# Routed expert items: where two steps of the second layer stand, and first-layer weights split in four pieces

## The chip, the cores and the metric

The kernel runs on one core of one Trainium2 chip. The metric is the device time of one execution in microseconds (us), from the program's first to its last instruction with what lies around it. Engines are named as the profile names them: PE is TensorE (PEld its weight loads), DVE is VectorE, ACT is ScalarE, POOL is GpSimd, SP is the engine that issues the large loads.

## The reference

Three parts follow one another: clustered attention, a mixture of eight experts in which every token goes to one expert, and a second, dense mixture whose eight experts see every token. The change touches the middle part only. N is 1536 tokens, D 512, F 1024, E 8 experts; everything is 32-bit floating point.

```
def _moe_ref(x, expert_emb, tau, w1, w2):
    xn = x / (norm(x) + 1e-06); en = expert_emb / (norm(expert_emb) + 1e-06)
    logits = xn @ en.T / tau
    expert_idx = argmax(logits, axis=1)
    probs = softmax(logits);  gate_w = probs[arange(N), expert_idx]
    for e in range(E):
        mask = expert_idx == e
        h = maximum(x[mask] @ w1[e], 0.0)          # first layer, relu
        out[mask] = gate_w[mask, None] * (h @ w2[e])   # second layer
```

## The kernel before

A product of 32-bit numbers is made from three faster ones. Each operand is split in a high part (fp32r, written by ACT, `split_hi`, line 877, the instruction at L879) and a low part (written by DVE, `split_lo`, line 882, the instruction at L884, which subtracts the high part from the operand). PE then adds high by high, high by low and low by high.

The routed part sorts the tokens by expert and cuts them in 19 items of 128 tokens; item n has one expert. Items 0 and 1 are written out (`tile(0, 0)`, `tile(0, 1)`), items 2 to 17 are a hardware loop of two items a turn, item 18 has a code of its own (`last_tile`) that also begins the dense part. Each engine runs its own program; what couples them are semaphores, and what stands in an engine's queue behind a waiting instruction waits with it.

For an item PE does this (`tile`, line 1253): the first layer's output half s = 0 in 12 products (lines 1267 to 1269), half s = 1 in 12 products with the four transposes of the first hidden half in their middle (`transpose_h(n, 0)`, L1217), then the four transposes of the next item's tokens (`transpose_x`, L1210), the four of the second hidden half (`transpose_h(n, 1)`, L1217), and the second layer in eight steps f = 0 to 7 of three products each (lines 1280 to 1282). Steps 0 to 3 read the first hidden half and the first half of w2, steps 4 to 7 the second halves.

Between them stand, for every item:

- ACT: `read_out` of the item before (L1528), the high part of the second half of w2 (`w2_part(.., 1)`), the relu of each hidden half (L1506), the high parts of the hidden halves (`h_part`), of the next tokens (`x_part`), of the next item's w1 in the pieces of `W1_PARTS`, and of the next item's first half of w2.
- DVE: the low parts of the same data: w2's second half, first hidden half, tokens, second hidden half, w1's pieces, w2's first half. It reads the item's expert number into a register ahead of w1's pieces (`expert_of`, L1801).
- POOL: adds the item before to the output rows (`add_rows`, L2167) and then gathers the tokens of the item after next with an indirect DMA (`gather`, L2124).
- SP: loads the raw weights of an expert a good item ahead of their use.

Weights are split anew for every item: w1 is 128 x 4096 numbers, w2 the same.

What the names in the profile are: `moe_bank` is PSUM; `all_w_hi`, `all_w_lo`, `all_w_raw` are w1; `moe_routed_w_hi`, `moe_routed_w_lo`, `moe_w_raw` are w2; `moe_h_rows` is the relu's output, `moe_routed_h_hi` and `moe_routed_h_lo` the transposed hidden halves; `moe_x_rows` the gathered tokens and `moe_x_hi`, `moe_x_lo` their transposes; `all_x` holds the output rows, `moe_y` one item's output.

Of the kernel before, what the change touches and what calls it, by code (L numbers as in the profile page):

```python
# [24 lines left out]
W1_PARTS = ((0, 2, 0), (2, 2, 0), (0, 4, 1))  # L25
# [155 lines left out]
def attention(nc, sems, c, made, q, k, v, centroids, expert_emb, tau, w1, X, L, xs, W1R, w1_loaded, x_stored):  # L181
# [7 lines left out]
    with ExitStack() as stack:  # L189
# [346 lines left out]
        def scalar(act, experts):  # L536
# [89 lines left out]
            experts.first_w1_hi(act, 2)  # L626
            copy_out_t(G // 2 - 1, 13)
# [277 lines left out]
def expert_layers(nc, sems, attn, c, X, L, w1, w2, xs, out_row, w_gate, dense_w1, dense_w2, out_dram, W1R, W1H, W1L,  # L905
                  w1_at, stationary_at, scratch_at, w1_loaded, x_stored):

    with ExitStack() as stack:
# [291 lines left out]
        def tensor(pe):  # L1200
# [52 lines left out]
            def tile(i, j):  # L1253
# [3 lines left out]
                for s in range(2):  # L1257
                    pe.wait_ge(w1_lo, 3 * n + s + 2)
# [14 lines left out]
                if not last:  # L1273
                    transpose_x(i + j, 1 - j)
                transpose_h(n, 1)
                for f in range(FC):
                    if f % 4 == 0:
                        pe.wait_ge(rh_lo, 2 * n + f // 4 + 1)
                        pe.wait_ge(rw2_lo, 2 * n + f // 4 + 1)
                    pe.matmul(ps_y[:], RHH[:, f, :], RW2H[:, f, :], start=(f == 0), stop=False)  # L1280
                    pe.matmul(ps_y[:], RHH[:, f, :], RW2L[:, f, :], start=False, stop=False)  # L1281
                    mm = pe.matmul(ps_y[:], RHL[:, f, :], RW2H[:, f, :], start=False, stop=(f == FC - 1))  # L1282
                    if f == 3:
                        mm.then_inc(w2_used, 1)
# [189 lines left out]
        def scalar(act):  # L1474
# [55 lines left out]
            def tile(i, j):  # L1530
# [13 lines left out]
                h_part(n, 0)  # L1544
                relu(n, 1)
                x_part(n + 1)
                h_part(n, 1)
                if first:
                    r = expert_of(n + 1)
                    w1_part(i + j, 1 - j, 0, r)  # L1550
                w1_part(i + j, 1 - j, 1, r)
                w1_part(i + j, 1 - j, 2, r)
# [205 lines left out]
        def vector(dve):  # L1758
# [44 lines left out]
            def w1_part(n, r, part):  # L1803
                dve.wait_ge(w1_hi, 3 * n + part + 1)
# [80 lines left out]
            def tile(i, j):  # L1885
# [4 lines left out]
                if first:  # L1890
                    sum_gates()
                    h_part(n, 0)
                    w2_part(n, 0, 1)
                else:
                    w2_part(n, expert_of(n), 1)
                    h_part(n, 0)
                x_part(n + 1)
                h_part(n, 1)
                if first:
                    find_gates()  # L1900
                r = expert_of(n + 1)
                w1_part(n + 1, r, 0)
                w1_part(n + 1, r, 1)
                w1_part(n + 1, r, 2)
# [194 lines left out]
            first_w1_lo(dve, 2)  # L2099
            w2_part(0, 0, 0)  # L2100
# [199 lines left out]
```

## Time and profile before

| | us |
|---|---|
| median of three runs | 1614.45 (1612.37 to 1615.25) |
| the profiled execution's own time | 1614.62 |
| its span | 1612.8 |
| granted clock of TensorE over the span | 0.994 |
| items 2 to 17 (351.47 to 557.01) | 16 times 12.85 |

The page of the profile gives PE 1578.4 us of busy time (98% of the span), DVE 1189.9 (74%), ACT 771.0 (48%), POOL 247.2 (15%). In the stretch of the routed items, which lies between 323 and 579 us, DVE stands near PE. A row of a timeline gives the start of an instruction in us, its duration in us, engine, line, operation, and in square brackets the idle time of the engine before it with what ended that idle time. Instructions of an engine overlap a little: the next DVE instruction starts some 0.08 us before the row's end of the one ahead, and a matmul's row lasts 0.39 us while the next one starts 0.23 us after it.

### The profile page before, as it was taken

The page shows a single profiled execution, that of the slowest core. Times are in us where ns is not written, and L with a number is a line of the kernel's source. Part 1 is how long each engine was busy: PE and PEld are TensorE (multiplying, and loading weights), DVE is VectorE, ACT ScalarE, POOL GpSimd, SP SyncE. Part 2 cuts the span into 40 slices and gives each one's busy share as a digit, 9 for nine tenths or more (in the row PEclk, how much of TensorE's full clock was granted, in tenths as well). Part 3 has the DMA queues.
Part 4 walks back from the last instruction along what each step waited for, and adds up shares of the span by engine and source line. Part 5 has one row for each costly group of instructions (what it writes and reads, how often), then busy time and mean ns, then how long its engine had stood idle before and what let it go on. Part 6 is the DMA issues. An engine that isn't in the chain of part 4 may idle for free.

```text
span 1612.8 us, 27116 instructions
## 1 busy us (share of the span) xinstructions
PE 1578.4 (98%) x8416; PEld 1397.6 (87%) x8416; DVE 1189.9 (74%) x2010; ACT 771.0 (48%) x1377; POOL 247.2 (15%) x314
## 2 busy tenths in 40 slices
PE   8999999899999989999999999999999999999998
PEld 7999999677777778898998989899898989989897
DVE  7999999999999974877665666656566665656664
ACT  5777779778888852322333233233323323222331
POOL 2111111213333350100010010001001000100102
PEclk8999999999999999999999999999999999999999
DMA  4223323354334310110010011001001100100002
GB/s 100 60 60 71 76 59 89 92 190 145 141 130 141 132 40 14 40 40 27 27 53 26 26 39 40 26 26 53 26 26 40 39 26 27 52 26 26 26 0 78
DMA packets 123699, 94.91 MB, mean 59 GB/s; under 512 B 66344, under 2 KB 101160, under 8 KB 123632
## 3 DMA queue, kind: packets, MB, share of 16 engines
q1 hardware_dynamic: 120848, 86.01, 17.7%
q0 software_dynamic: 2480, 8.13, 1.7%
q8 instruction: 21, 0.34, 0.1%
q14 instruction: 46, 0.38, 0.1%
q10 hardware_dynamic: 304, 0.05, 0.0%
HBM read 87.88 MB, written 6.29 MB: 58 GB/s over the span
## 4 chain that ended last, share of the span: by engine, by line
PE 88%; DVE 7%; issue 3%; ACT 2%; DMA 0%; DVEq 0%; SPq 0%; POOL 0%; ACTq 0%; POOLq 0%
PE moe_bank L1346 11%; PE moe_bank L1344 11%; PE moe_bank L1345 11%; PE moe_bank L1321 10%; PE moe_bank L1324 10%; PE moe_bank L1323 10%; PE attn_ps_out L441 2%; PE moe_bank L1267 2%; PE moe_bank L1269 2%; PE moe_bank L1268 2%; PE attn_ps_probs_t L422 2%; PE moe_bank L1280 2%; PE moe_bank L1282 2%; PE moe_bank L1281 2%; PE attn_ps_prep L347 1%
## 5 line engine op out<-in xcount | busy, mean ns | idle before, releaser
L1968 DVE SCALAR_TENSOR_TENSOR all_x<-moe_bank,all_x 128x512 f32<-128x512 f32 x336 | 251.3, 748 | 129.1 <-PE moe_bank L1346 126.4
L1321 PE MATMUL moe_bank<-moe_x_t_hi,all_w_hi 128*128 128x384 f32 x896 | 305.1, 341 | 3.0 <-DVE all_w_lo L884 2.9
L1324 PE MATMUL moe_bank<-moe_x_t_hi,all_w_lo 128*128 128x384 f32 x896 | 303.2, 338 | 0.0
L1323 PE MATMUL moe_bank<-moe_x_t_lo,all_w_hi 128*128 128x384 f32 x896 | 302.3, 337 | 0.0
L1344 PE MATMUL moe_bank<-moe_w_hi,moe_h_hi 128*128 128x512 f32 x768 | 301.1, 392 | 0.0
L1345 PE MATMUL moe_bank<-moe_w_lo,moe_h_hi 128*128 128x512 f32 x768 | 300.8, 392 | 0.0
L1346 PE MATMUL moe_bank<-moe_w_hi,moe_h_lo 128*128 128x512 f32 x672 | 265.0, 394 | 0.0
L1321 PEld LDWEIGHTS moe_bank<-moe_x_t_hi,all_w_hi 128*128 128x128 f32 x896 | 168.6, 188 | 14.0 <-issue 3.6
L1323 PEld LDWEIGHTS moe_bank<-moe_x_t_lo,all_w_hi 128*128 128x128 f32 x896 | 168.6, 188 | 11.3
L1324 PEld LDWEIGHTS moe_bank<-moe_x_t_hi,all_w_lo 128*128 128x128 f32 x896 | 168.5, 188 | 0.0
L1345 PEld LDWEIGHTS moe_bank<-moe_w_lo,moe_h_hi 128*128 128x128 f32 x768 | 144.2, 188 | 22.4
L1344 PEld LDWEIGHTS moe_bank<-moe_w_hi,moe_h_hi 128*128 128x128 f32 x768 | 144.4, 188 | 21.8
L2129 POOL TENSOR_TENSOR moe_w_sums<-moe_dense_w_raw 128x256 f32<-128x256 f32 x32 | 23.7, 740 | 853.0 <-DVE all_w_lo L884 853.0
L1346 PEld LDWEIGHTS moe_bank<-moe_w_hi,moe_h_lo 128*128 128x128 f32 x672 | 126.0, 188 | 28.6
L1676 ACT ACTIVATE moe_h_hi<-all_x 128x384 fp32r<-128x384 f32 x63 | 33.2, 526 | 169.4 <-DVE all_x L2077 169.4
L1648 ACT ACTIVATE moe_h_hi<-moe_p 128x384 fp32r<-128x384 f32 x63 | 33.2, 526 | 147.0 <-DVE moe_p L2036 147.0
L2036 DVE TENSOR_TENSOR moe_p<-moe_bank,moe_p 128x384 f32<-128x384 f32 x63 | 35.1, 557 | 90.7 <-PE moe_bank L1324 80.2
L884 DVE TENSOR_TENSOR moe_routed_w_lo<-moe_w_raw,moe_routed_w_hi 128x2048 fp32r<-128x2048 f32 x38 | 98.7, 2598 | 4.5 <-ACT moe_routed_w_hi L879 3.7
L637 DVE TENSOR_TENSOR attn_probs_t_lo<-attn_ps_probs_t,attn_probs_t_hi 128x384 fp32r<-128x384 f32 x192 | 97.1, 546 | 2.4 <-ACT attn_probs_t_hi L564 1.3
L1669 ACT ACTIVATE moe_h_hi<-moe_bank 128x384 fp32r<-128x384 f32 x63 | 31.0, 492 | 134.6 <-PE moe_bank L1324 134.6
L691 DVE CUSTOM_DVE_ANT_0 attn_scores<-attn_ps_scores,attn_mask 128x768 f32<-128x768 f32 x96 | 91.1, 949 | 2.6 <-issue 0.6
L558 ACT ACTIVATE attn_probs<-attn_scores,attn_row_max 128x768 f32<-128x768 f32 x96 | 91.3, 951 | 3.2 <-DVE attn_row_max L691 3.1
(325 smaller groups left out, 3065.7 us busy)
## 6 DMA issues: line engine op xcount, KB each, us to landing
all_w_raw<-in_moe_w SPq DMA_DIRECT2D x8, 2048.0 KB, 7.5
moe_w_raw<-in_moe_w SPq DMA_DIRECT2D x8, 2048.0 KB, 9.2
moe_dense_w_raw<-in_moe_w SPq DMA_DIRECT2D x64, 256.0 KB, 3.1
moe_dense_w_raw<-in_moe_w SPq DMA_DIRECT2D x32, 512.0 KB, 3.3
attn_q_raw<-in_q SPq DMA_DIRECT2D x32, 192.0 KB, 3.4
attn_k_raw<-in_k SPq DMA_DIRECT2D x32, 192.0 KB, 3.8
attn_v_raw<-in_v SPq DMA_DIRECT2D x16, 192.0 KB, 3.8
tokens<-all_x SPq DMA_DIRECT2D x32, 96.0 KB, 2.0
```

Source lines behind the costliest of these rows:

```text
L558: act.activation(PR[s % 2][:], SM[s % 2][:], ACT.Exp, bias=MX[s % 2][:], scale=-1.0, accum_out=SUM[:, s % 12:s % 12 + 1]).then_inc(exp_don ...
L637: return dve.tensor_tensor(out, src, hi.bitcast(F32), ALU.subtract)
L691: dve.tensor_tensor_reduce(out=SM[s % 2][:].rearrange("p (a k) -> p a k", a=2), in0=ps_s[s % 2][:, :, 0:3 * P], in1=MASK[s % 2][:].rearran ...
L884: return dve.tensor_tensor(out, src, hi.bitcast(F32), ALU.subtract)
L1321: pe.matmul(out, hi[:, s, k, :], XH[chunk][:, x, k, :], start=(start and k == 0), stop=False, skip_group_check=True)
L1323: pe.matmul(out, hi[:, s, k, :], XL[chunk][:, x, k, :], start=False, stop=False, skip_group_check=True)
L1324: mm = pe.matmul(out, lo[:, s, k, :], XH[chunk][:, x, k, :], start=False, stop=(stop and k == 1), skip_group_check=True)
L1344: pe.matmul(out, HH[h][hidden][:, rows], W2H[j][:, f, :], start=(f == 0), stop=False)
L1345: pe.matmul(out, HH[h][hidden][:, rows], W2L[j][:, f, :], start=False, stop=False)
L1346: mm = pe.matmul(out, HL[h][hidden][:, rows], W2H[j][:, f, :], start=False, stop=(f == 1))
L1968: dve.scalar_tensor_tensor(acc, y, PROB[:, row, bass.ds(at, 1)], acc, ALU.mult, ALU.add).then_inc(y_added, 1)
L2036: dve.tensor_tensor(CP1[:], m, CP1[:], ALU.add).then_inc(summed, 1)
```

## The change

In PE's queue the first two steps of the second layer (f = 0, 1) come ahead of the transposes of the second hidden half, and these ahead of the transposes of the next tokens; item 18 has the first of these moves too. w1 is split in four pieces of 128 x 1024 in place of two of 128 x 1024 and one of 128 x 2048, also for the first weights, which are prepared during the attention part. From item 1 on, DVE makes the first two of these pieces between the two hidden halves, then the second hidden half, the tokens and the other two pieces; ACT makes the pieces 1 and 2 on either side of the second relu, and the second hidden half ahead of the tokens. The semaphore counts follow (four pieces an item).

```diff
--- before.py
+++ after.py
@@ -22,7 +22,7 @@
 DC, FC = D // P, F // P
 ITEMS = NT + E - 1
 FOLD = DH + E
-W1_PARTS = ((0, 2, 0), (2, 2, 0), (0, 4, 1))
+W1_PARTS = ((0, 2, 0), (2, 2, 0), (0, 2, 1), (2, 2, 1))
 ROUNDS = 8
 
 
@@ -624,6 +624,7 @@
             for s in range(2, 12):
                 step(G // 2 - 1, s)
             experts.first_w1_hi(act, 2)
+            experts.first_w1_hi(act, 3)
             copy_out_t(G // 2 - 1, 13)
 
         def rank(engine, done):
@@ -1255,7 +1256,7 @@
                 last = last_of(i, j)
                 pe.wait_ge(rx_lo, n + 1)
                 for s in range(2):
-                    pe.wait_ge(w1_lo, 3 * n + s + 2)
+                    pe.wait_ge(w1_lo, 4 * n + 2 * s + 2)
                     if first_of(i) and j == 1 and s == 1:
                         find_gates()
                     for k in range(DC):
@@ -1270,10 +1271,11 @@
                     mm.then_inc(h_ready, 1)
                     if last:
                         transpose_pair(2 * s)
-                if not last:
-                    transpose_x(i + j, 1 - j)
-                transpose_h(n, 1)
                 for f in range(FC):
+                    if f == 2:
+                        transpose_h(n, 1)
+                        if not last:
+                            transpose_x(i + j, 1 - j)
                     if f % 4 == 0:
                         pe.wait_ge(rh_lo, 2 * n + f // 4 + 1)
                         pe.wait_ge(rw2_lo, 2 * n + f // 4 + 1)
@@ -1542,14 +1544,18 @@
                     act.wait_ge(found, SCALED)
                     read_out(0, 0)
                 h_part(n, 0)
+                if not first:
+                    w1_part(i + j, 1 - j, 1, r)
                 relu(n, 1)
+                if not first:
+                    w1_part(i + j, 1 - j, 2, r)
+                h_part(n, 1)
                 x_part(n + 1)
-                h_part(n, 1)
                 if first:
                     r = expert_of(n + 1)
-                    w1_part(i + j, 1 - j, 0, r)
-                w1_part(i + j, 1 - j, 1, r)
-                w1_part(i + j, 1 - j, 2, r)
+                    for part in range(3):
+                        w1_part(i + j, 1 - j, part, r)
+                w1_part(i + j, 1 - j, 3, r)
                 w2_part(i + j, 1 - j, 0, r)
                 if not first:
                     if not first_of(i):
@@ -1801,7 +1807,7 @@
                 return dve.value_load(expert[0:1, bass.ds(n, 1)], min_val=0, max_val=E - 1)
 
             def w1_part(n, r, part):
-                dve.wait_ge(w1_hi, 3 * n + part + 1)
+                dve.wait_ge(w1_hi, 4 * n + part + 1)
                 chunk, chunks, s = W1_PARTS[part]
                 cols = slice(s * 512, (s + 1) * 512)
                 split_lo(dve, W1L[:, chunk:chunk + chunks, cols], W1R[:, bass.ds((r % 2) * DC + chunk, chunks), cols],
@@ -1891,17 +1897,22 @@
                     sum_gates()
                     h_part(n, 0)
                     w2_part(n, 0, 1)
+                    h_part(n, 1)
+                    x_part(n + 1)
+                    find_gates()
+                    r = expert_of(n + 1)
+                    for part in range(4):
+                        w1_part(n + 1, r, part)
                 else:
                     w2_part(n, expert_of(n), 1)
                     h_part(n, 0)
-                x_part(n + 1)
-                h_part(n, 1)
-                if first:
-                    find_gates()
-                r = expert_of(n + 1)
-                w1_part(n + 1, r, 0)
-                w1_part(n + 1, r, 1)
-                w1_part(n + 1, r, 2)
+                    r = expert_of(n + 1)
+                    w1_part(n + 1, r, 0)
+                    w1_part(n + 1, r, 1)
+                    h_part(n, 1)
+                    x_part(n + 1)
+                    w1_part(n + 1, r, 2)
+                    w1_part(n + 1, r, 3)
                 w2_part(n + 1, r, 0)
                 if first:
                     dve.wait_ge(gates_found, 1)
@@ -2097,6 +2108,7 @@
             shift_logits()
             x_part(0)
             first_w1_lo(dve, 2)
+            first_w1_lo(dve, 3)
             w2_part(0, 0, 0)
             turns(dve, tile)
             first_unit()
```

PE's queue in a loop item, from the last product of the first layer on, before (`moe_h_relu` is the relu of a hidden half, `moe_x_loaded` a gather's landing, `moe_routed_w2_lo` and `moe_routed_h_lo` are DVE's low parts):

```order
L1269 MATMUL moe_bank<-all_w_hi,moe_x_lo 128x512
L1210 MATMUL moe_bank<-all_ident,moe_x_rows 128x128 [waits moe_x_loaded0]
L1210 MATMUL moe_bank<-all_ident,moe_x_rows 128x128 x3
L1217 MATMUL moe_bank<-all_ident,moe_h_rows 128x128 [waits moe_h_relu]
L1217 MATMUL moe_bank<-all_ident,moe_h_rows 128x128 x3
L1280 MATMUL moe_bank<-moe_routed_w_hi,moe_routed_h_hi 128x512 [waits moe_routed_w2_lo,moe_routed_h_lo]
L1281 MATMUL moe_bank<-moe_routed_w_lo,moe_routed_h_hi 128x512
L1282 MATMUL moe_bank<-moe_routed_w_hi,moe_routed_h_lo 128x512
L1280 MATMUL moe_bank<-moe_routed_w_hi,moe_routed_h_hi 128x512
```

and now, from the same product on (line numbers are one or two higher):

```order
L1270 MATMUL moe_bank<-all_w_hi,moe_x_lo 128x512
L1282 MATMUL moe_bank<-moe_routed_w_hi,moe_routed_h_hi 128x512 [waits moe_routed_w2_lo,moe_routed_h_lo]
L1283 MATMUL moe_bank<-moe_routed_w_lo,moe_routed_h_hi 128x512
L1284 MATMUL moe_bank<-moe_routed_w_hi,moe_routed_h_lo 128x512
L1282 MATMUL moe_bank<-moe_routed_w_hi,moe_routed_h_hi 128x512
L1283 MATMUL moe_bank<-moe_routed_w_lo,moe_routed_h_hi 128x512
L1284 MATMUL moe_bank<-moe_routed_w_hi,moe_routed_h_lo 128x512
L1218 MATMUL moe_bank<-all_ident,moe_h_rows 128x128 [waits moe_h_relu]
L1218 MATMUL moe_bank<-all_ident,moe_h_rows 128x128 x3
L1211 MATMUL moe_bank<-all_ident,moe_x_rows 128x128 [waits moe_x_loaded0]
L1211 MATMUL moe_bank<-all_ident,moe_x_rows 128x128 x3
L1282 MATMUL moe_bank<-moe_routed_w_hi,moe_routed_h_hi 128x512
```

The two steps and their wait for DVE's low parts stand in front of both groups of transposes, which now follow one another.

DVE's queue in a loop item, from the second half of w2 on, before (rows that only compute a register are left out):

```order
L884 TENSOR_TENSOR moe_routed_w_lo<-moe_w_raw,moe_routed_w_hi 128x2048
L884 TENSOR_TENSOR moe_routed_h_lo<-moe_bank,moe_routed_h_hi 128x512 [waits moe_routed_h_hi]
L884 TENSOR_TENSOR moe_x_lo<-moe_bank,moe_x_hi 128x512 [waits moe_routed_x_hi]
L884 TENSOR_TENSOR moe_routed_h_lo<-moe_bank,moe_routed_h_hi 128x512 [waits moe_routed_h_hi]
L884 ISA [waits moe_w1_hi_done]
L884 TENSOR_TENSOR all_w_lo<-all_w_raw,all_w_hi 128x2x512
L884 ISA [waits moe_w1_hi_done]
L884 TENSOR_TENSOR all_w_lo<-all_w_raw,all_w_hi 128x2x512
```

and now:

```order
L885 TENSOR_TENSOR moe_routed_w_lo<-moe_w_raw,moe_routed_w_hi 128x2048
L885 TENSOR_TENSOR moe_routed_h_lo<-moe_bank,moe_routed_h_hi 128x512 [waits moe_routed_h_hi]
L885 ISA [waits moe_w1_hi_done]
L885 TENSOR_TENSOR all_w_lo<-all_w_raw,all_w_hi 128x2x512
L885 ISA [waits moe_w1_hi_done]
L885 TENSOR_TENSOR all_w_lo<-all_w_raw,all_w_hi 128x2x512
L885 TENSOR_TENSOR moe_routed_h_lo<-moe_bank,moe_routed_h_hi 128x512 [waits moe_routed_h_hi]
L885 TENSOR_TENSOR moe_x_lo<-moe_bank,moe_x_hi 128x512 [waits moe_routed_x_hi]
L885 ISA [waits moe_w1_hi_done]
L885 TENSOR_TENSOR all_w_lo<-all_w_raw,all_w_hi 128x2x512
L885 ISA [waits moe_w1_hi_done]
L885 TENSOR_TENSOR all_w_lo<-all_w_raw,all_w_hi 128x2x512
```

The item's order on DVE is now: first hidden half, two pieces of w1, second hidden half, tokens, two pieces of w1. What stands ahead of the first hidden half, w2's second half with its wait for ACT, has not moved.

## Rows read from the trace of the kernel before

**Rows 1.** Busy time of each engine over the stretch of items 2 to 17: us, PE, PEld, DVE, ACT, POOL.
```profile
351.00:557.00 206.00, 201.99 (x963) 163.85 (x962) 188.70 (x129) 175.31 (x177) 73.42 (x31) 1.00 0.42 147
```

**Rows 2.** Timeline of PE in items 8 and 9: start, us, line, operation.
```profile
428.55 0.40 PE L1267 MATMUL moe_bank<-all_w_hi,moe_x_hi 128*128 128x512 f32 x1
...
434.35 0.39 PE L1269 MATMUL moe_bank<-all_w_hi,moe_x_lo 128*128 128x512 f32 x1
...
435.43 0.66 PE L1217 MATMUL moe_bank<-all_ident,moe_h_rows 128*128 128x128 f32 x4 [0.25 <-ACT moe_h_rows L1506]
...
436.15 0.39 PE L1281 MATMUL moe_bank<-moe_routed_w_lo,moe_routed_h_hi 128*128 128x512 f32 x1
...
441.40 0.40 PE L1267 MATMUL moe_bank<-all_w_hi,moe_x_hi 128*128 128x512 f32 x1
```

**Rows 3.** Timeline of DVE in the same two items.
```profile
432.19 2.83 DVE L884 TENSOR_TENSOR moe_routed_w_lo<-moe_w_raw,moe_routed_w_hi 128x2048 fp32r<-128x2048 f32 x1 [0.48 <-ACT moe_routed_w_hi L879]
434.94 0.68 DVE L884 TENSOR_TENSOR moe_routed_h_lo<-moe_bank,moe_routed_h_hi 128x512 fp32r<-128x512 f32 x1
...
436.75 0.69 DVE L884 TENSOR_TENSOR moe_routed_h_lo<-moe_bank,moe_routed_h_hi 128x512 fp32r<-128x512 f32 x1 [0.16 <-ACT moe_routed_h_hi L879]
437.80 1.23 DVE L884 TENSOR_TENSOR all_w_lo<-all_w_raw,all_w_hi 128x1024 fp32r<-128x1024 f32 x1 [0.36 <-ACT all_w_hi L879]
...
442.28 2.28 DVE L884 TENSOR_TENSOR moe_routed_w_lo<-moe_w_raw,moe_routed_w_hi 128x2048 fp32r<-128x2048 f32 x1
444.64 3.22 DVE L884 TENSOR_TENSOR moe_routed_w_lo<-moe_w_raw,moe_routed_w_hi 128x2048 fp32r<-128x2048 f32 x1
```

**Rows 4.** Timeline of ACT, the second half of the second-layer weights.
```profile
430.03 1.92 ACT L879 ACTIVATE moe_routed_w_hi<-moe_w_raw 128x2048 fp32r x1 [0.45 <-issue]
...
442.48 1.92 ACT L879 ACTIVATE moe_routed_w_hi<-moe_w_raw 128x2048 fp32r x1
```

**Rows 5.** Timeline of POOL, items 8 and 9, then item 1.
```profile
430.89 1.97 POOL L2167 TENSOR_TENSOR all_x<-all_x,moe_y 128x512 f32 x1 [7.90 <-issue]
433.02 2.83 POOL L2124 DMA_INDIRECT moe_x_rows<-tokens,moe_token_of_item  x1 [0.15 <-POOL all_x L2167]
444.11 1.61 POOL L2167 TENSOR_TENSOR all_x<-all_x,moe_y 128x512 f32 x1 [8.26 <-issue]
...
344.98 1.27 POOL L2167 TENSOR_TENSOR all_x<-all_x,moe_y 128x512 f32 x1 [22.05 <-issue]
346.40 0.96 POOL L2124 DMA_INDIRECT moe_x_rows<-tokens,moe_token_of_item  x1
```

**Rows 6.** Timeline of DVE and PE where item 1 starts.
```profile
335.29 2.36 DVE L884 TENSOR_TENSOR all_w_lo<-all_w_raw,all_w_hi 128x1024 fp32r<-128x1024 f32 x2 [0.51 <-issue]
337.80 0.47 PE L1267 MATMUL moe_bank<-all_w_hi,moe_x_hi 128*128 128x512 f32 x1 [1.37 <-DVE all_w_lo L884]
```

**Rows 7.** Timeline of PE, eight transposes and what follows (item 18).
```profile
562.43 1.06 PE L1238 MATMUL moe_bank<-all_ident,moe_token_sums 128*128 128x128 f32 x8 [1.80 <-POOL moe_token_sums L2159]
563.25 0.48 PE L1267 MATMUL moe_bank<-all_w_hi,moe_x_hi 128*128 128x512 f32 x1
563.56 0.39 PE L1268 MATMUL moe_bank<-all_w_lo,moe_x_hi 128*128 128x512 f32 x1
```

**Rows 8.** Timeline of DVE in item 0.
```profile
328.95 0.69 DVE L884 TENSOR_TENSOR moe_routed_h_lo<-moe_bank,moe_routed_h_hi 128x512 fp32r<-128x512 f32 x1 [0.59 <-ACT moe_routed_h_hi L879]
...
332.95 0.16 DVE L1876 CAST moe_gate_part<-moe_gate 128x12 bf16<-128x12 f32 x1
```

**Rows 9.** Timeline of DVE and PE in item 1.
```profile
344.61 0.68 DVE L884 TENSOR_TENSOR moe_routed_h_lo<-moe_bank,moe_routed_h_hi 128x512 fp32r<-128x512 f32 x1
...
346.21 0.39 PE L1281 MATMUL moe_bank<-moe_routed_w_lo,moe_routed_h_hi 128*128 128x512 f32 x1
```

**Rows 10.** Timeline of PE behind its longest wait.
```profile
594.75 0.41 PE L1321 MATMUL moe_bank<-moe_x_t_hi,all_w_hi 128*128 128x384 f32 x1 [2.94 <-DVE all_w_lo L884]
...
596.61 0.52 PE L1321 MATMUL moe_bank<-moe_x_t_hi,all_w_hi 128*128 128x384 f32 x1
```

## The prediction

> **What bounds the kernel now.** I read the page first (PE busy 98% of the span, so only what lies on PE's own path can move the time), then the busy time by stretch, then the timelines of PE, DVE, ACT and POOL over two neighbouring loop items. In the stretch of items 2 to 17 DVE is busy 188.7 of 206 us and PE 202.0 [rows 1]: two engines near their limit. An item lasts 441.40 - 428.55 = 12.85 us [rows 2], and the 16 items of the loop are alike.
>
> I count times in an item from its first product (T = 428.55 for item 8, 441.40 for item 9). The last product of the first layer starts at 5.80. Then come the eight transposes, and the second product of the second layer starts at 7.60 [rows 2]: 1.80 us. Eight transposes without a gap take less: 0.23 to the first of them, 0.82 for the eight, 0.31 from the first product behind them to the second [rows 7], together 1.36. The missing 0.44 us is the hole in which PE waits for the relu; its row shows 0.25 of it as idle, the rest is the pipeline's emptying. That hole is what the change can remove: 16 x 0.44 = 7.0 us.
>
> The other side is what the first two steps need: DVE's low part of the first hidden half, which stands behind DVE's low part of w2's second half. It ends at 434.94 + 0.68 = 435.62 in item 8, T + 7.07, and at the same place in item 9 (444.64 + 3.22 = 447.86 ends w2, and the hidden half follows as in item 8) [rows 3]. PE could start the second layer at T + 6.03, so today these low parts come one microsecond too late for the new place; the transposes cover that now.
>
> **When the low part will be ready.** Call its end E. What sets it is w2's second half on DVE, so I take that apart.
>
> - ACT's high part of it ends at T + 3.40 in even items (430.03 + 1.92) and T + 3.00 in odd ones (442.48 + 1.92) [rows 4]. It cannot come earlier, since it waits for the item before to end and for its read-out. DVE begins 0.24 behind it (432.19 against 431.95) [rows 3, 4]: T + 3.64 and T + 3.24.
> - DVE's own queue is later than that now (w2's first half runs at T + 0.88 to 3.16 in item 9, 442.28 + 2.28 [rows 3]). With the new order it will not be: below, w2's first half ends near T + 2.0.
> - POOL's addition. It starts at T + 2.34 (430.89), lasts 1.97 there, but 1.27 in item 1, where DVE leaves it alone [rows 5]. In item 9 DVE's w2 starts at 444.64, takes 3.22 instead of 2.28, and ends 2.14 behind the addition's end (444.11 + 1.61 = 445.72); in item 8 it ends 435.02, 2.16 behind 432.86 [rows 3, 5]. So the two do not overlap: whichever comes second does its work behind the other. The Trainium skill says the same (SBUF — State Buffer, section Who interferes with whom): a DVE instruction with two inputs in SBUF and a GpSimd instruction that reads SBUF exclude one another for a whole instruction, and the loser waits. By that rule, which these rows bear out, the estimate for an odd item is the later one of the two that follow; if the two engines only overlapped freely, it would be the earlier one.
> - With DVE idle at T + 2.34 the addition runs alone and ends at T + 2.34 + 1.27 = 3.61. Odd items: DVE is blocked from 3.24 to 3.61, needs 2.15 more, 5.76; the hidden half starts 0.08 ahead of that row's end and lasts 0.68: E = T + 6.36. Even items: DVE starts at 3.64, lasts 2.28: E = 3.64 + 2.28 - 0.08 + 0.68 = T + 6.52. Without the blocking the odd ones would have E = 3.24 + 2.88 = T + 6.12.
>
> **The new item.** Behind a DVE end PE's first product starts 0.15 later (335.29 + 2.36 = 337.65 against 337.80 [rows 6]) and the second 0.31 after it, as behind transposes [rows 7]: E + 0.46. Today 5.25 us lie between the second product and the next item (441.40 - 436.15 [rows 2]), 23 spacings of 0.228. New: four spacings to the end of step 1 (0.91), 1.36 for the eight transposes up to the second product behind them, 17 spacings (3.88). So the item lasts E + 0.46 + 0.91 + 1.36 + 3.88 = E + 6.61. It breaks even at E = 6.24, and it is over that in both kinds: 12.97 in odd items, 13.13 in even ones, mean 13.05, against 12.85. That is +0.20 x 16 = **+3.2 us** where -7 was to be had.
>
> Is anything else later than E? The second hidden half: its transposes start at E + 1.37 + 0.23 = E + 1.60. Now it takes 436.75 - 435.43 = 1.32 from their start to DVE's low part [rows 2, 3], which gives E + 2.92, end E + 3.60, and 0.15 to PE: E + 3.75. Step 4 wants it at E + 0.46 + 0.91 + 1.36 + 5 x 0.228 = E + 3.87. It just fits. DVE is free for it: behind the first hidden half come 0.36 for reading the expert (437.80 row) and two pieces of w1, 2.36 in one row of two [rows 3, 6], to about E + 2.64. Then tokens (0.61), two pieces (2.28) and w2's first half (2.2) end near E + 2.92 + 0.61 + 0.61 + 2.28 + 2.2 = E + 8.62, which is T + 2.01 of the next item. So DVE has some 1 us of slack an item and the w1 pieces are ready ahead of their use. Splitting the 128 x 2048 piece costs 2.36 - 2.28 = 0.08 on DVE and lies in that slack; in the attention part it comes once, and I put 0.1 there.
>
> **Items 0, 1 and 18.** Item 0 keeps DVE's w1 pieces behind the gates. E = 328.95 + 0.69 = 329.64 [rows 8]. Its tokens now come last: second hidden half E + 2.92, tokens start E + 3.53 and are followed by the next piece at about E + 4.1 = 333.7 instead of 332.95 [rows 8]. Item 1 starts when DVE has done two w1 pieces [rows 6], so it starts 0.8 later: **+0.8**.
>
> Item 1: E = 344.61 + 0.68 = 345.29 and the second product at 346.21 [rows 9] comes at 345.75, -0.46; then two spacings (0.46) turn into 1.36, +0.90: together +0.44. Besides, w1's pieces now stand where POOL's addition (344.98 to 346.25) and the gather (346.40, 0.96) run [rows 5]. The first piece wants 345.65 and gets 346.25, ends 347.4; the gather, waiting since 346.40, goes ahead of the second piece to about 348.3, that ends at 349.5, the second hidden half at 350.1. With 0.15 and a restart of 0.08 that is 1.1 behind the 349.2 at which step 4 wants it. Bounds 0 and 1.1; the gather in item 8 waited (2.83 against 0.96 [rows 5]) until DVE was done and then got its turn, so I take 1.1: **+1.5**.
>
> Item 18 has no tokens to transpose but loses the cover for its second hidden half and switches between the two kinds of product once more (0.08). I bound it by 0 and 0.8 and take **+0.4**.
>
> **Sum.** 1614.62 (the profiled execution, 0.17 above the median of the runs) + 3.2 + 0.8 + 1.5 + 0.4 + 0.1 = 1620.6; against the median 1620.4. I forecast **1620.4 us**, 0.4% slower.
>
> **The rivals.**
>
> 1. It works as the order suggests: DVE, rid of its backlog, delivers by T + 5.9 and nothing waits. Then 16 x 0.44 = 7.0 us go and items 0, 1 and 18 cost some 1: 1608.6. For it speaks that E falls by 0.6 us in any case; against it the ACT rows, after which 2.88 us of DVE work remain [rows 4]. It decides from E below 6.24. Chance 0.08.
> 2. The addition does not block DVE in odd items, and the gather does not come between w1's pieces: odd items 12.73, mean 12.93, +1.3; items 0, 1 and 18 +1.6: 1617.4. Against it the two rows that end 2.14 and 2.16 behind an addition. Chance 0.24, counted with other small savings on PE's restart (each 0.1 us is 1.6 us).
> 3. The gather wins against w2's second half. It will start at T + 3.61 + 0.15 = 3.76, and DVE in even items at 3.64, only 0.12 ahead. If it loses, E rises by about 1.0 in eight items: 1620.4 + 8 = 1628. For it: the narrow margin; against it: DVE is still the first to ask. Chance 0.10.
> 4. TensorE's clock. Before item 1 PE will be idle for about 2.1 us (now 1.37 [rows 6]). Behind the idle 2.94 us at 594.75 the same product goes from 0.34 to 0.52 us [rows 10]; if that happens here, with half the clock over some 3 us, add 2: 1622.4. Chance 0.08.
>
> The forecast itself has 0.50.
>
> **How the numbers follow.** Faster by over 0.2% (below 1611.2) needs rival 1: 0.08, and 0.01 for the rest. Within 0.2% (1611.2 to 1617.7; about what a measurement of this kernel can tell from no change) holds rival 2: 0.24. Slower: 0.50 + 0.10 + 0.08 less the 0.01: 0.67. The range from 1614 to 1627 leaves out rival 1 and most of rival 3, and holds an error of 0.4 us an item in E downwards and upwards.
>
> **What the next profile would show.** Right: items of 12.9 to 13.2 us; PE waits ahead of the first L1282 for DVE's moe_routed_h_lo in every loop item, 0.3 to 0.6 us; no wait for the relu; the addition lasts 1.3 us instead of 1.97; w2's second half on DVE starts at T + 3.2 and 3.6; DVE's w2 first half ends near T + 2; item 1 starts 0.8 us later. Wrong: items under 12.8 and no wait at L1282 (rival 1); odd items 0.4 shorter than even ones, with DVE's w2 at 2.28 us (rival 2); DVE's w2 above 3 us behind a gather (rival 3); products of 0.5 us and more in item 1 (rival 4). A wait at step 4 in the loop items would show that the 0.12 us that I found there were not there.

## The result and the profile after

| | before | after |
|---|---|---|
| median of 20 runs each (us) | 1613.01 (1610.27 to 1615.25) | 1617.86 (1613.86 to 1620.64) |
| ratio | 1 | 1.0028, interval 1.0022 to 1.0035 |
| span of the profiled execution | 1612.8 | 1617.2 |

The changed kernel is 4.85 us slower; 5.95 had been forecast over the median known then. The changed kernel was later profiled a second time, which helps to part what the change does from what differs between executions:

| stretch (us) | before | after | after, second profile |
|---|---|---|---|
| start to item 0 | 323.32 | 321.32 | 320.99 |
| item 0 | 14.48 | 14.83 | 14.84 |
| item 1 | 13.67 | 15.56 | 14.19 |
| items 2 to 17 | 205.54 | 208.31 | 208.23 |
| item 18 to the first dense product | 21.75 | 21.04 | 21.04 |
| dense part to the end | 1034.1 | 1036.1 | 1034.8 |

The loop carries +2.7 us in both profiles of after, 0.17 an item. That is the answer to the question that the prediction asked.

Two rows of the table need care. The first, 2.0 and 2.3 us shorter, is not the change: the granted clock of the first 40 us is 0.87 in the profile of before and 0.91 in both of after, and experiment 2, whose attention part is that of before, has 0.91 too and starts item 0 at 321.47. And the 0.7 us that the fifth row gains are given back in the sixth, where PE waits for DVE, in before and after:

```profile
587.63 0.85 PE L1238 MATMUL moe_bank<-all_ident,all_x 128*128 128x128 f32 x6 [0.38 <-DVE moe_x_t_lo L884]
```
```profile
590.60 0.85 PE L1239 MATMUL moe_bank<-all_ident,all_x 128*128 128x128 f32 x6 [1.06 <-DVE moe_x_t_lo L885]
597.72 0.66 PE L1323 MATMUL moe_bank<-moe_x_t_hi,all_w_hi 128*128 128x384 f32 x1 [2.94 <-DVE all_w_lo L885]
```

The product behind PE's longest wait starts 37.74 us behind the start of item 18 in before (594.75 [rows 10]) and 37.70 in both profiles of after.

Timeline of PE of the changed kernel, item 8 and the start of item 9 (L1282 to L1284 are the second layer, L1218 and L1211 the transposes; compare [rows 2]):

```profile
429.71 0.40 PE L1268 MATMUL moe_bank<-all_w_hi,moe_x_hi 128*128 128x512 f32 x1
...
435.52 0.40 PE L1270 MATMUL moe_bank<-all_w_hi,moe_x_lo 128*128 128x512 f32 x1
436.31 0.50 PE L1282 MATMUL moe_bank<-moe_routed_w_hi,moe_routed_h_hi 128*128 128x512 f32 x1 [0.39 <-DVE moe_routed_h_lo L885]
436.64 0.39 PE L1283 MATMUL moe_bank<-moe_routed_w_lo,moe_routed_h_hi 128*128 128x512 f32 x1
...
437.80 0.60 PE L1218 MATMUL moe_bank<-all_ident,moe_h_rows 128*128 128x128 f32 x4
438.23 0.60 PE L1211 MATMUL moe_bank<-all_ident,moe_x_rows 128*128 128x128 f32 x4
...
442.80 0.40 PE L1268 MATMUL moe_bank<-all_w_hi,moe_x_hi 128*128 128x512 f32 x1
```

The wait for the relu ahead of the transposes is gone; a longer one for DVE's low part stands ahead of the second layer. The item lasts 13.09 us. What DVE and POOL do in items 8 and 9 (compare [rows 3, 5]):

```profile
433.36 2.29 DVE L885 TENSOR_TENSOR moe_routed_w_lo<-moe_w_raw,moe_routed_w_hi 128x2048 fp32r<-128x2048 f32 x1 [1.60 <-ACT moe_routed_w_hi L880]
435.57 0.68 DVE L885 TENSOR_TENSOR moe_routed_h_lo<-moe_bank,moe_routed_h_hi 128x512 fp32r<-128x512 f32 x1
436.37 2.36 DVE L885 TENSOR_TENSOR all_w_lo<-all_w_raw,all_w_hi 128x1024 fp32r<-128x1024 f32 x2
439.07 0.69 DVE L885 TENSOR_TENSOR moe_routed_h_lo<-moe_bank,moe_routed_h_hi 128x512 fp32r<-128x512 f32 x1 [0.34 <-ACT moe_routed_h_hi L880]
...
446.06 2.90 DVE L885 TENSOR_TENSOR moe_routed_w_lo<-moe_w_raw,moe_routed_w_hi 128x2048 fp32r<-128x2048 f32 x1 [1.24 <-ACT moe_routed_w_hi L880]
```
```profile
432.06 1.29 POOL L2179 TENSOR_TENSOR all_x<-all_x,moe_y 128x512 f32 x1 [8.64 <-issue]
433.50 2.98 POOL L2136 DMA_INDIRECT moe_x_rows<-tokens,moe_token_of_item  x1
445.52 1.29 POOL L2179 TENSOR_TENSOR all_x<-all_x,moe_y 128x512 f32 x1 [9.03 <-issue]
446.95 2.84 POOL L2136 DMA_INDIRECT moe_x_rows<-tokens,moe_token_of_item  x1
```

DVE now waits 1.60 and 1.24 us for ACT's high part of w2; before it waited 0.48 in item 8 and, late by its own queue, not at all in item 9. Its low part of the first hidden half ends at T + 6.54 in item 8. The waits of the stretch from 323 to 585 us (us in total, times, longest) name the new releaser:

```profile
DVE moe_routed_w_lo L885 <- ACT moe_routed_w_hi L880: 22.2, 16, 1.6
...
PE moe_bank L1282 <- DVE moe_routed_h_lo L885: 6.0, 17, 0.6
```

Busy time of the loop, of item 1 in two pieces, and of a stretch in the dense part's start (us, then PE, PEld, DVE, ACT, POOL, granted clock, DMA share, GB/s; compare [rows 1]):

```profile
351.71:560.02 208.31, 202.86 (x961) 162.53 (x960) 178.56 (x145) 174.80 (x192) 64.27 (x31) 1.00 0.42 145
336.15:339.50 3.35, 3.35 (x11) 2.69 (x12) 3.35 (x3) 2.74 (x2) 0.00 (x0) 0.73 0.49 188
339.50:341.10 1.60, 1.60 (x23) 1.08 (x23) 0.98 (x1) 0.60 (x1) 0.00 (x0) 0.50 0.00 0
...
597.00:604.00 7.00, 6.28 (x20) 6.27 (x21) 3.03 (x5) 1.96 (x3) 4.16 (x4) 0.51 0.29 92
```

DVE is 10 us less busy in the loop, mostly because the addition no longer holds its w2 part for long (2.29 us in even items and 2.54 in odd ones, 2.83 and 3.22 before), and the loop is slower all the same: busy time was not the bound, the order was.

### The profile page after: what moved, and what is told of

Same layout as the page of the kernel before. It is cut to its first block, busy times and chain, and to the rows that moved or that the text cites. A ratio compares the mean times of both kernels' runs of the same rounds, so it can differ in the third digit from the quotient of the medians.

```text
span 1617.2 us, 27199 instructions
## 1 busy us (share of the span) xinstructions
PE 1582.1 (98%) x8416; PEld 1397.5 (86%) x8416; DVE 1181.7 (73%) x2029; ACT 771.7 (48%) x1396; POOL 239.2 (15%) x314
## 4 chain that ended last, share of the span: by engine, by line
PE 82%; DVE 8%; issue 4%; ACT 3%; DMA 1%; DVEq 1%; ACTq 1%; SPq 0%; POOL 0%
PE moe_bank L1348 11%; PE moe_bank L1346 11%; PE moe_bank L1347 11%; PE moe_bank L1323 10%; PE moe_bank L1326 10%; PE moe_bank L1325 10%; PE attn_ps_out L441 3%; PE moe_bank L1282 2%; PE attn_ps_probs_t L422 2%; PE moe_bank L1284 2%; PE moe_bank L1283 2%; ACT moe_routed_w_hi L880 2%; DVE moe_routed_w_lo L885 1%; PE attn_ps_scores L411 1%; PE attn_ps_scores L412 1%
## 5 line engine op out<-in xcount | busy, mean ns | idle before, releaser
L885 DVE TENSOR_TENSOR moe_routed_w_lo<-moe_w_raw,moe_routed_w_hi 128x2048 fp32r<-128x2048 f32 x38 | 89.3, 2351 | 22.8 <-ACT moe_routed_w_hi L880 22.2
```

Of the source, the lines that this page charges most:

```text
L885: return dve.tensor_tensor(out, src, hi.bitcast(F32), ALU.subtract)
```

## The experiments

T is an item's first product and E the end of DVE's low part of the first hidden half, as in the prediction. Ratios are to the kernel before, measured beside each.

**1. PE's order alone undone** (the rest of the change stays).

```diff
+                if not last:
+                    transpose_x(i + j, 1 - j)
+                transpose_h(n, 1)
                 for f in range(FC):
-                    if f == 2:
-                        transpose_h(n, 1)
-                        if not last:
-                            transpose_x(i + j, 1 - j)
```

> The changed kernel with PE's queue as it was before (tokens, then second hidden half, then the second layer), all else as changed: four pieces of w1 and the new order on ACT and DVE. Theory A (the loss is the cover that the transposes gave to DVE's low part of the first hidden half): that low part still ends near T + 6.4 and 6.5 in a loop item, but PE is not there before T + 7.29, so loop items last 12.85 us as before; only item 1 loses up to 0.7 us. Time 0 to 1 us above the kernel before (ratio 1.000 to 1.0006). Theory B (the loss is in the pieces and in DVE's and ACT's new order): the loss stays, ratio 1.002 to 1.003.

Measured 1615.32 us, ratio 1.0013 (1.0004 to 1.0022). The time is 2.25 us above before, over the 0 to 1 us expected, and the items are 13.04, not 12.85. PE waits for the second relu again, and longer than before (it was 4.0 us over 16 waits between 340 and 545 us in the kernel before, 0.3 at most):

```profile
PE moe_bank L1218 <- ACT moe_h_rows L1507: 7.1, 16, 0.7
```

The new order of ACT has a piece of w1 ahead of that relu, which starts at T + 6.43 instead of T + 6.23. I had overlooked that part of the change; the new place of PE's steps hides it. Experiment 2 shows the other half, experiment 3 tests this reading.

**2. PE's order alone done** (kernel before, with PE's lines of the change and nothing else: the diff above read the other way).

> The kernel before with the change in PE's queue alone; three pieces of w1, ACT and DVE in their old order. Theory A: DVE now meets the tokens and the second hidden half with nothing to do in between, idle about 3.3 us behind the first hidden half, and its w1 and w2 pieces come after, so DVE sets the item: I work out a cycle of 3.3 + 0.6 + 0.6 + 0.4 + 4.5 + 2.2 + 1.15 (POOL's addition) + 2.15 + 0.6 = 15.5 us an item, +2.7 each, some +40 us, ratio near 1.025. Theory B: without the new pieces and order the move costs nothing or gains, ratio 0.996 to 1.000.

Measured 1675.24 us, ratio 1.0387 (1.0372 to 1.0403). The first loop items last 15.4 to 15.5 us, as worked out; from item 8 on they last 17.05. The busy time of the items ahead of and behind that point (columns as above) and three neighbouring products show why:

```profile
367.32:421.00 53.68, 45.16 (x209) 34.96 (x207) 43.20 (x27) 37.98 (x40) 20.61 (x8) 1.00 0.29 102
445.55:600.00 154.45, 132.18 (x546) 102.77 (x545) 108.61 (x73) 97.32 (x101) 48.13 (x18) 0.90 0.31 106
```
```profile
455.75 0.63 PE L1283 MATMUL moe_bank<-moe_routed_w_hi,moe_routed_h_lo 128*128 128x512 f32 x1
456.18 1.05 PE L1217 MATMUL moe_bank<-all_ident,moe_h_rows 128*128 128x128 f32 x4
...
458.05 0.40 PE L1283 MATMUL moe_bank<-moe_routed_w_hi,moe_routed_h_lo 128*128 128x512 f32 x1
```

Each item from item 8 on, and item 6, has a stretch of 3.4 us at half the clock (1.2 GHz: 0.63 us a product instead of 0.40). These stretches cost 1.6 us each, some 16 of the 62 us; the rest is DVE's order. So the reordering on ACT and DVE is not a nicety: without it the same move of PE costs 62 us in place of 5.

**3. PE's order undone, and the relu ahead of the piece of w1.**

```diff
-                if not first:
-                    w1_part(i + j, 1 - j, 1, r)
                 relu(n, 1)
                 if not first:
+                    w1_part(i + j, 1 - j, 1, r)
                     w1_part(i + j, 1 - j, 2, r)
```

> a1_pe_undone (changed kernel, PE in its old order) with ACT's second relu ahead of the w1 piece that the change had put in front of it. Theory: that piece, high part 1.06 us long, holds the relu back from T + 6.23 to T + 6.43 and this alone made the loop items 13.04 us in a1_pe_undone; with the relu first they last 12.85 us as in the kernel before. Rival: the 0.2 us come from DVE's order or the fourth piece, and items stay at 13.04.

One execution: 1612.84 us, relu at T + 6.23, items 12.87. The 0.17 us of experiment 1 are ACT's order.

**4. The addition taken away** (POOL writes zeros instead, for items 2 to 16; their outputs are left out).

```diff
+                if 2 <= n < ITEMS - 2:
+                    pool.memset(OUTZ[:, NT, :], 0.0).then_inc(ry_added, 1)
+                else:
                     pool.tensor_tensor(OUT[:, bass.ds(t, 1), :] ... ALU.add).then_inc(ry_added, 1)
```

> The changed kernel in which POOL, for items 2 to 16, writes zeros to a row of its own in place of adding the item's output to the output rows (those outputs are left out): same semaphores, but POOL reads nothing there. Without the addition nothing keeps DVE from starting w2's second half at T + 3.25 in odd items. If the gather, which then starts about T + 3.0, does not hold DVE up when it is first: odd items E = T + 6.12, 12.65 us (now 12.91), even items unchanged at 13.09. If the gather holds DVE up like the addition does: DVE is blocked to about T + 4.0, E near T + 6.7, and items of both kinds last about 13.3 us. If POOL has no part in it at all: 12.91 and 13.09 as now.

One execution: 1613.7 us. Odd items last 12.80 to 12.87 instead of 12.91, even ones 13.05 as before. DVE, POOL and ACT in item 9 (T = 440.88):

```profile
444.14 2.29 DVE L885 TENSOR_TENSOR moe_routed_w_lo<-moe_w_raw,moe_routed_w_hi 128x2048 fp32r<-128x2048 f32 x1 [1.22 <-ACT moe_routed_w_hi L880]
446.49 0.69 DVE L885 TENSOR_TENSOR moe_routed_h_lo<-moe_bank,moe_routed_h_hi 128x512 fp32r<-128x512 f32 x1
```
```profile
444.11 0.95 POOL L2136 DMA_INDIRECT moe_x_rows<-tokens,moe_token_of_item  x1 [0.49 <-POOL all_x L2180]
```
```profile
444.91 1.06 ACT L880 ACTIVATE all_w_hi<-all_w_raw 128x1024 fp32r x1 [0.44 <-issue]
445.88 0.58 ACT L880 ACTIVATE moe_routed_h_hi<-moe_bank 128x512 fp32r<-128x512 f32 x1
```

Two things. Without the addition w2's low part is 2.29 us, so in after the addition does hold it (2.54 to 2.90 in odd items). But E falls only to T + 6.31 and not to 6.12: DVE then waits for ACT's high part of the hidden half (445.88 + 0.58 = T + 5.58), which stands behind a piece of w1. The addition costs 0.08 us an odd item; a second chain lies right under the first. And the gather, which here starts 0.03 us ahead of DVE's w2 (0.4 to 0.8 in the other items from 3 on), lasts 0.95 us and DVE 2.29: neither holds the other. In after, where it starts behind DVE, it lasts 2.83 to 3.04.

**5. Ten warm-up products ahead of item 1** (`warm(10)` at the head of item 1 on PE).

> The changed kernel with ten more matmuls of 512 columns (of ones, result not read) on PE between items 0 and 1, where PE idles 1.8 us. Theory A (the idle time lets the clock fall in item 1, where products last 0.63 us for 3.4 us): the products of item 1 stay at 0.39 us, item 1 lasts about 14.3 us instead of 15.56, and the time falls by 1 to 1.3 us against the changed kernel (ratio to before 1.002). Rival (the fall of the clock has nothing to do with this idle time): item 1 unchanged.

Measured 1616.69 us, ratio 1.0022 (1.0012 to 1.0031); item 1 lasts 14.31 and runs at full clock. That looked like the proof, but experiment 4, with the same idle time ahead of item 1 (1.82 us), had no slow stretch there either. So the changed kernel was profiled again:

> The changed kernel itself, profiled once more, for one question: in its first profile item 1 runs 3.4 us at half the clock and lasts 15.56 us, while two kernels with the same idle time ahead of item 1 show no such stretch there (14.20 and 14.23 us). If the idle time decides it, item 1 reads 15.5 again. If it depends on the run, item 1 can read 14.2 to 14.3 here. Items of the loop 12.91 and 13.08 as before either way.

1615.92 us, item 1 at 14.19. The same stretch of the same program, here at full clock (compare with the two rows of item 1 above):

```profile
335.83:339.50 3.67, 3.67 (x37) 2.95 (x38) 3.67 (x3) 3.34 (x3) 0.00 (x0) 1.00 0.45 172
339.50:341.10 1.60, 1.60 (x10) 1.29 (x10) 1.56 (x4) 1.33 (x2) 0.00 (x0) 1.00 0.00 0
```

The slow stretch in item 1 comes in some executions of one program and not in others. It costs 1.4 us when it comes. Of five profiles with 1.7 to 1.8 us of idle time ahead of item 1 two have it (the first of after, and experiment 9; not the second of after, nor experiments 2 and 4); none of the six with 1.0 to 1.4 us has it (before, experiments 1, 3, 6, 7 and 8). That speaks for rival 4's link and does not settle it; of the two kernels that the expectation names with the same idle time, experiment 1 turned out to have only 1.02 us.

**6. The split of w1 alone** (kernel before with four pieces, all orders as they were).

```diff
-W1_PARTS = ((0, 2, 0), (2, 2, 0), (0, 4, 1))
+W1_PARTS = ((0, 2, 0), (2, 2, 0), (0, 2, 1), (2, 2, 1))
...
-                    pe.wait_ge(w1_lo, 3 * n + s + 2)
+                    pe.wait_ge(w1_lo, 4 * n + 2 * s + 2)
...
-                w1_part(i + j, 1 - j, 1, r)
-                w1_part(i + j, 1 - j, 2, r)
+                for part in range(1, 4):
+                    w1_part(i + j, 1 - j, part, r)
```

> The kernel before with only w1 split in four pieces (128 x 1024 each), every order as before. The prediction's term for this part is 0.1 us, and nothing an item, because DVE and ACT have the room. If that holds: items of the loop 12.85 us, item 1 13.7, time within 0.5 us of the kernel before (ratio 0.9997 to 1.0003, which with the spread of the runs can read 0.999 to 1.001). Rival: four pieces cost an instruction's start more on DVE (0.08 us) and on ACT in every item, and DVE stands near its limit there; if that reaches PE, the items are 12.93 and the time is 1.3 us above before.

Measured 1614.6 us, ratio 1.0011 (1.0001 to 1.0020). Loop items 12.85, item 1 13.67, as expected. Not expected: item 0 is 0.36 shorter (14.12), and item 18 up to the first dense product 1.94 longer (23.69). Item 0: DVE starts w1 0.14 us behind the gates, not 0.51 as in [rows 6]; what takes that time away is open:

```profile
332.00 1.01 DVE L1883 TENSOR_TENSOR moe_item_gates<-moe_item_one_hot,moe_gate_part 128x228 bf16<-128x228 bf16 x3
333.15 3.50 DVE L885 TENSOR_TENSOR all_w_lo<-all_w_raw,all_w_hi 128x1024 fp32r<-128x1024 f32 x3
```

Item 18: PE's transposes of the token sums wait 4.77 us for POOL, 1.80 before [rows 7], and behind that wait PE has 3.4 us at half the clock, which before has nowhere in item 18; the eight transposes last 1.50 us instead of 1.06:

```profile
563.26 1.50 PE L1239 MATMUL moe_bank<-all_ident,moe_token_sums 128*128 128x128 f32 x8 [4.77 <-POOL moe_token_sums L2160]
```
```profile
563.70:567.20 3.50, 3.50 (x13) 2.82 (x12) 1.38 (x2) 1.19 (x2) 2.85 (x5) 0.51 0.00 0
```
```profile
558.50 3.81 POOL L2157 TENSOR_TENSOR moe_token_sums<-all_x,moe_token_sums 128x256 f32<-128x256 f32 x1 [12.09 <-DVE moe_token_sums L1830]
562.39 0.72 POOL L2160 TENSOR_TENSOR moe_token_sums<-all_x,moe_token_sums 128x256 f32<-128x256 f32 x1
```
```profile
558.34 0.41 DVE L1832 TENSOR_TENSOR moe_token_sums<-all_x 128x256 f32<-128x256 f32 x1
558.68 0.41 DVE L1830 TENSOR_TENSOR moe_token_sums<-all_x 128x256 f32<-128x256 f32 x1
559.01 0.41 DVE L1832 TENSOR_TENSOR moe_token_sums<-all_x 128x256 f32<-128x256 f32 x1
559.35 0.18 DVE L885 TENSOR_TENSOR moe_w_gate_hi_lo<-moe_w_gate_raw,moe_w_gate_hi_lo 128x32 fp32r<-128x32 f32 x1
559.45 2.28 DVE L885 TENSOR_TENSOR moe_routed_w_lo<-moe_w_raw,moe_routed_w_hi 128x2048 fp32r<-128x2048 f32 x1
```

POOL's sum needs 0.72 us alone. Here DVE wins four short instructions in a row and then the long one, and POOL's ends 0.58 behind it. In before and after the two take turns: DVE's same sums last 0.42, 0.42, 0.95, 0.94, and POOL's second sum is done in time. The same code, shifted by a fraction of a microsecond, makes PE wait 3 us more. What the item is longer by, 1.94, holds also the stretch at half the clock (up to 1.7, half of its 3.4, by estimate), and three later waits for DVE that before has there (0.83, 0.88 and 0.59) are gone. How much of the 1.94 each makes is open. The ten executions of this kernel have a mean granted clock of 0.9926, against 0.9942 for before beside them, so a slow stretch more is the rule here and not one profile's accident. The two stretches together make +1.6 us, and the medians differ by 1.4.

**7. A better order: the tokens' transposes first, then step 0, then the second hidden half, then steps 1 to 7** (ACT and DVE make their parts in that order).

```diff
                 for f in range(FC):
-                    if f == 2:
+                    if f == 0 and not last:
+                        transpose_x(i + j, 1 - j)
+                    if f == 1:
                         transpose_h(n, 1)
-                        if not last:
-                            transpose_x(i + j, 1 - j)
```

> The changed kernel with another order: PE transposes the tokens, then step 0 of the second layer, then the second hidden half, then steps 1 to 7; ACT takes the tokens right behind the second relu, DVE the tokens behind one w1 piece, then the second hidden half, then the other three pieces. If the low part of the first hidden half (E = T + 6.4 and 6.5) is what PE waits for, four transposes of tokens (0.44 us) cover nearly all of it: second product at about T + 6.9, loop items 6.9 + 0.91 + 2 x 0.44 + ... = 12.5 to 12.6 us, 16 x 0.3 = 4 to 5 us under the kernel before (ratio 0.997). If something else sets the item (DVE's total work, the gather against the w1 pieces), items stay at 12.9 or more.

Measured 1608.16 us, ratio 0.9973 (0.9963 to 0.9982), items 12.49 and 12.63. The four token transposes cover most of the wait for E (in even items step 0 starts at T + 6.60; in experiment 8, where nothing is waited for, at T + 6.38), and step 0 covers the wait for the relu.

**8. The same, with ACT's w2 part ahead of the read-out.**

```diff
                 if not first:
                     w2_part(i, j, 1, expert_of(n))
+                if not first_of(i):
+                    act.wait_ge(ry_added, n - 1)
+                    read_out(n - 1, 1 - j)
                 relu(n, 0)
...
                 w2_part(i + j, 1 - j, 0, r)
-                if not first:
-                    if not first_of(i):
-                        act.wait_ge(ry_added, n)
-                    read_out(n, j)
```

> As b1_tokens_first, and ACT makes the high part of w2's second half ahead of the read-out of the item before, in place of behind it. ACT then ends it at about T + 2.3 in place of 3.0 and 3.4. By the theory that two chains meet at the first hidden half (w2's low part, and ACT's own high part of the hidden half, ready at T + 5.6), E falls to T + 6.3 in every item and no further: items 0.1 to 0.2 us under those of b1_tokens_first. POOL's addition starts near T + 4.2 and now collides with DVE's w2 the other way round (POOL waits). Rival: the addition and the gather, one microsecond later, hold up DVE's w1 pieces and through them the second hidden half, and items are longer than in b1_tokens_first.

Measured 1605.41 us, ratio 0.9957 (0.9943 to 0.9970): the fastest of all, 7.7 us under the kernel before. Items last 12.39 to 12.43 from item 3 on, and the loop row has PE busy for its whole length:

```profile
349.45:548.18 198.73, 198.73 (x962) 162.61 (x960) 177.54 (x145) 173.96 (x193) 43.12 (x31) 1.00 0.44 152
```

The loop is 6.8 us shorter than before (198.73 against 205.54): nearly all of the 7.0 that the prediction had put on the hole. DVE's w2 part now starts at T + 2.55, ahead of the addition, which waits (1.82 us from T + 4.17) and holds nobody:

```profile
426.70 2.29 DVE L885 TENSOR_TENSOR moe_routed_w_lo<-moe_w_raw,moe_routed_w_hi 128x2048 fp32r<-128x2048 f32 x1 [0.23 <-ACT moe_routed_w_hi L880]
429.77 0.69 DVE L885 TENSOR_TENSOR moe_routed_h_lo<-moe_bank,moe_routed_h_hi 128x512 fp32r<-128x512 f32 x1 [0.78 <-ACT moe_routed_h_hi L880]
```

**9. The changed kernel with that ACT order alone.**

> The changed kernel with that one move on ACT (high part of w2's second half ahead of the read-out), PE and DVE as changed. Theory: E goes from T + 6.40 and 6.54 to T + 6.31 in all loop items, items last 12.85 us, 2.4 us less over the 16 (ratio to before 1.0013). If ACT's high part of w2 were not what sets E in even items, they stay at 13.09.

Measured 1614.08 us, ratio 1.0009 (1.0000 to 1.0018); E = T + 6.30 to 6.33 and items of 12.80 to 12.86 from item 3 on (item 2: 6.55 and 13.10). With E at 6.31 the item is E + 6.5, at the old length: PE's order of the change only breaks even there, as the prediction's 6.24 said within 0.1.

## Why the prediction was right, and where it wasn't

- **The hole of 0.44 and what replaces it: right.** It disappeared, and PE waits instead for E, in every loop item, up to 0.6 us. E was forecast at T + 6.36 and 6.52; it is 6.39 to 6.41 and, in most even items, 6.54. The items were to last 12.97 and 13.13; they last 12.91 and 13.09, so the loop term is +2.8 instead of +3.2. The item is E + 6.51 to 6.55 and not E + 6.61, mostly because PE's restart was put at 0.46 and is 0.39 (in item 8 from 436.25, the end of DVE's row, to 436.64, the second product).
- **The addition: right in its length (1.29, forecast 1.27), and in that it holds DVE.** In item 9, where it starts 0.4 later, E is 6.76. But the E = 6.12 of rival 2 was not to be had: experiment 4 shows ACT's high part of the hidden half as the next limit, at E = 6.31. I had taken w2's part for the only chain.
- **The second hidden half fits: right**, by the margin found: no wait at step 4 in the loop. DVE's slack of 1 us is there; it waits 1.24 to 1.60 for ACT.
- **Item 0: the mechanism right, one effect missed.** The order costs 0.71 (14.83 against 14.12 with the split alone; forecast 0.8). The split gives back 0.36, which I had not foreseen.
- **Item 1: the term of 1.1 us failed.** It said that the first piece of w1 would wait for the addition and that the gather would then hold up the second. The first half came: the piece takes 2.14 us in the second profile of after. The second didn't. The gather waited for the end of the first piece and ran on beside the second, which was not stretched:

```profile
344.44 1.78 POOL L2136 DMA_INDIRECT moe_x_rows<-tokens,moe_token_of_item  x1
```
```profile
343.25 2.14 DVE L885 TENSOR_TENSOR all_w_lo<-all_w_raw,all_w_hi 128x1024 fp32r<-128x1024 f32 x1
345.31 1.21 DVE L885 TENSOR_TENSOR all_w_lo<-all_w_raw,all_w_hi 128x1024 fp32r<-128x1024 f32 x1
```

  The gather ends at 346.22, 0.83 behind the first piece's end and 0.30 ahead of the second's. Without a slow clock item 1 is 0.52 longer, near the first part of the term (+0.44). I had read from item 8 that a waiting gather gets its turn at the end of the DVE instruction ahead of it, which holds, and had charged DVE for that turn, which no row showed.
- **Rival 4 happened as well, in one of two profiles**: 1.4 us in item 1 at half the clock (forecast 2). So the forecast +1.5 for item 1 stands beside a measured +1.9 for other reasons.
- **Item 18: +0.4 forecast, nothing measured.** Up to the first dense product it is 0.7 shorter: PE's wait for POOL's sums fell from 1.80 to 0.71, which outweighs the new wait at step 4. But DVE's queue is not faster there (its first weights of the dense part start 18.04 us behind the item's start in before and after), so PE waits 0.7 longer a little later, as the rows above show. Experiment 1 has the product behind the longest wait at 36.58 instead of 37.74: PE's order costs 1.1 us in item 18, and the rest of the change gives as much. By experiment 6 the same stretch can move by 2 us through the turns of DVE and POOL and what the clock does behind them; no row of before could tell which.
- **The sum.** Parts that both profiles of after show: 0.36 (item 0) + 0.52 (item 1 at full clock) + 2.7 (loop) + 0 (item 18 with its give-back) = +3.6 us, against a forecast of 6.0. The medians differ by 4.85, with an interval of 3.5 to 5.6. The rest, some 1.2 us, fits the clock: the mean granted clock is 0.9936 over the 20 executions of after and 0.9941 to 0.9944 over those of before that stand beside the experiments, which is an estimated 0.9 to 1.4 us more lost to half the clock. In the profiles such stretches stand in item 1 (once in two) and near 597 (6.8 us in the first profile of after, 3.4 in the second and in before; this is 1.4 of the dense part's +2.1). So the forecast came this near partly by luck: every term of the sum was too large, by 2.4 us together (the 0.1 for the split in the attention part shows in no profile), and stretches of slow clock, which rival 4 had at a chance of 0.08 and the sum not at all, made up about half of it.

## What to carry over

Before PE's work is moved ahead, compute when each operand of its new place is ready, from the queue of the engine that makes it, and look for the second chain right under the first. Work that has its inputs long before (here the transposes of the next tokens) belongs where the wait is, instead of the work that needs the latest result. A move on one engine and the reordering of its suppliers have to be made together: alone they gave +62 and +2 us, together +5, and with the right piece in the gap -8.

## What the runs showed of the hardware

- DVE's subtraction with both inputs in SBUF and a gather of POOL: the gather that starts behind it lasts 2.83 to 3.04 us and ends 0.83 behind DVE's end; one that starts 0.03 to 0.8 ahead lasts 0.95, and DVE isn't stretched (2.29; 14 items of experiment 4). The exclusion that holds for the addition in both directions holds for the gather in one only, and only for the DVE instruction that runs when it starts: in item 1 it ended beside the next one. The Trainium skill (SBUF — State Buffer, section Who interferes with whom) names the read side as what such a DVE instruction shares; that would fit a gather that reads its indices at its start, which was not tested alone. The trace agrees on the inputs: beside the hidden half, which has one input in PSUM (434.94, 0.68 us in [rows 3]), the gather of item 8 ran on and ended.
- With short instructions of both engines side by side, who gets the turn isn't fixed: DVE's sums of 0.42 us went 0.42, 0.42, 0.95, 0.94 in two kernels, and four at 0.41 or 0.42 in a third, where POOL's sum took 3.81 instead of 0.72.
- Half the clock came and went within one program: in item 1 in one of two profiles, near 597 us for 6.8 us or 3.4. Behind the wait of 4.77 us in experiment 6 it came for 3.4 us; behind the 1.80 at the same place in before it didn't. In experiment 2 it came in every item from item 8 on, but in only one of the items 2 to 7, though these waited as long.
